# Twelve attention chunks ahead of two expert layers: the first four chunks in halves of 64 tokens

## The reference

```python
# q, k, v: (2, 8, 768, 64), block = 64
for b in range(nb):
    intra = np.einsum('bhic,bhjc->bhij', qb, kb) * Dmask[None]
    intra = np.einsum('bhij,bhjd->bhid', intra, vb)
    inter = np.einsum('bhid,bhde->bhie', qb * lam_pow[None], kv_state)
    out[:, :, sl] = intra + inter
    kb_dec = kb * rev_pow[None]
    kv_state = lam_block * kv_state + np.einsum('bhsd,bhse->bhde', kb_dec, vb)
x = out as (1536, 512)
h = x @ w_in;  g = np.maximum(0.01 * h, h);  x = g @ w_out
...
```

## Time and profile before

| | |
|---|---|
| median of 3 runs | 473.35 us (473.17 to 473.56) |
| the profiled execution: its own time | 473.61 us |
| its span, first to last instruction | 471.9 us |
| TensorE busy | 464.3 us, 98% of the span |
| VectorE, ScalarE, GpSimd busy | 42%, 36%, 43% |
| TensorE's share of the chain that ended last | 97% |
| first dense matmul starts | 21.50 us |
| mean rate of the DMA engines | 112 GB/s |

### The profile page before, as it was taken

One profiled execution on the slowest core, in us unless ns is written; L12 is line 12 of the kernel. 1 busy time (PEld: TensorE's weight loads), 2 busy tenths in 40 slices (PEclk: granted clock), 3 DMA queues, 4 the chain that ended last, 5 costly groups with the idle time before them and its releaser, 6 DMA issues.

```text
span 471.9 us, 9883 instructions
## 1 busy us (share of the span) xinstructions
PE 464.3 (98%) x3622; PEld 385.9 (82%) x3623; DVE 198.1 (42%) x467; ACT 168.9 (36%) x291; POOL 202.9 (43%) x207
## 2 busy tenths in 40 slices
PE   8899999999999999999999999999999999999996
PEld 5777777777778888887788888889999999999965
DVE  5643433344365522222472255668531455131212
ACT  2244334434453444444444465552111343111110
POOL 6875456455424456644444576513112325030102
PEclk9999999999999999999999999999999999999999
DMA  8884554430030450000760000131117878821101
GB/s 313 290 278 150 180 179 139 150 113 13 1 88 3 147 209 0 0 0 1 198 249 0 1 1 11 35 94 42 45 46 229 288 243 266 255 87 32 46 2 44
DMA packets 31185, 52.71 MB, mean 112 GB/s; under 512 B 8833, under 2 KB 19201, under 8 KB 31154
## 3 DMA queue, kind: packets, MB, share of 16 engines
q1 hardware_dynamic: 25808, 45.24, 29.5%
q0 software_dynamic: 2624, 7.03, 4.5%
q10 hardware_dynamic: 2722, 0.02, 0.3%
HBM read 45.87 MB, written 6.60 MB: 111 GB/s over the span
## 4 chain that ended last, share of the span: by engine, by line
PE 97%; DVE 1%; issue 1%; ACT 0%; POOL 0%; POOLq 0%; DVEq 0%
PE psum L1675 10%; PE psum L1685 9%; PE psum L1677 9%; PE psum L1676 9%; PE psum L1687 9%; PE psum L1686 9%; PE psum L1756 5%; PE psum L1757 5%; PE psum L1758 5%; PE psum L1772 5%; PE psum L1774 5%; PE psum L1773 5%; PE psum L1892 1%; PE psum L1520 1%; PE psum L1741 1%; PE psum L1619 1%
## 5 line engine op out<-in xcount | busy, mean ns | idle before, releaser
L677 POOL TENSOR_TENSOR wi_lo<-wd_raw,wi_hi 128x512 fp32r<-128x512 f32 x48 | 61.8, 1288 | 128.5 <-ACT wi_hi L863 128.4
L1675 PE MATMUL psum<-xT,wi_lo 128*128 128x512 f32 x192 | 77.4, 403 | 0.3 <-DVE xT L1113 0.3
L1685 PE MATMUL psum<-act_lo,wo_hi 128*128 128x512 f32 x192 | 75.7, 394 | 0.2 <-DVE act_lo L1176 0.2
L1677 PE MATMUL psum<-xT,wi_hi 128*128 128x512 f32 x192 | 75.0, 390 | 0.0
L1687 PE MATMUL psum<-act_hi,wo_hi 128*128 128x512 f32 x192 | 74.8, 390 | 0.0
L1676 PE MATMUL psum<-xT,wi_hi 128*128 128x512 f32 x192 | 74.8, 389 | 0.0
L1686 PE MATMUL psum<-act_hi,wo_lo 128*128 128x512 f32 x192 | 74.7, 389 | 0.0
L1173 DVE SCALAR_TENSOR_TENSOR act_f<-psum,act_f 128x512 f32<-128x512 f32 x48 | 33.1, 689 | 78.7 <-ACT act_f L884 78.3
L682 POOL TENSOR_TENSOR wo_lo<-wd_raw,wo_hi 128x512 fp32r<-128x512 f32 x48 | 61.9, 1290 | 4.1 <-ACT wo_hi L868 4.1
L884 ACT ACTIVATE act_f<-psum 128x512 f32<-128x512 f32 x48 | 28.7, 597 | 88.5 <-PE psum L1677 88.5
L1756 PE MATMUL psum<-xe_lo,we_hi 128*128 128x256 f32 x192 | 54.5, 284 | 0.0
(11 more groups left out here) (240 smaller groups left out, 735.8 us busy)
## 6 DMA issues: line engine op xcount, KB each, us to landing
we_raw<-w_exp SPq DMA_DIRECT2D x40, 512.0 KB, 5.3
qk_in<-attn_qk SPq DMA_DIRECT2D x10, 512.0 KB, 4.3
kv_in<-attn_kv SPq DMA_DIRECT2D x10, 512.0 KB, 3.3
wd_raw<-w_dense SPq DMA_DIRECT2D x16, 256.0 KB, 3.2
x_d<-x_r SPq DMA_DIRECT2D x12, 256.0 KB, 3.9
wd_raw<-w_dense SPq DMA_DIRECT2D x16, 128.0 KB, 2.9
wd_raw<-w_dense SPq DMA_DIRECT2D x32, 64.0 KB, 2.8
qk_more<-attn_qk SPq DMA_DIRECT2D x2, 512.0 KB, 5.7
```

The lines of the kernel that those rows point to most:

```text
L677: nc.gpsimd.tensor_tensor(wi_lo[:, r, :], dense_raw(f, 0), wi_hi[:, r, :].bitcast(F32), ALU.subtract).then_inc(s_wil, 1)
L1675: nc.tensor.matmul(h, w_lo, hi, start=(c == 0), stop=False)
L1677: mm = nc.tensor.matmul(h, w_hi, hi, start=False, stop=(c == DC - 1))
L1685: nc.tensor.matmul(bank(ACC + c), hi, act_lo[:, r, :], start=first, stop=False)
```

## The change

Chunks 0 to 3 take the half form too. What follows from that, engine by engine:

- **TensorE**: the old functions for whole chunks go. `early_scores`, `early_updates`, `early_values` and `early_state_part` are the half form, with a chunk's scores and then its output in the same two banks (`FIRST`) and updates in banks 6 and 7. The values come first and the state part adds to them; the second half of the values waits for the first half (`s_ho`). Chunk 0 has a state part for its second half alone. Seven warm-up matmuls stand in three places. The first `layer1` takes all products of the high parts first (`first_layer1`). The scores and updates of chunk 4 stand behind it.
- **VectorE**: mask and query decay of 64 columns; one operation per chunk for `probs`; a middle state (`early_middle`) and a next state of four small operations (`next_state`). The constants of the expert stage move behind the first pair of chunks.
- **ScalarE**: four products for the decayed state per chunk, which GpSimd made in one; the copies of the half mask go.
- **GpSimd**: key decay ahead of query decay; no state products; one more select in the setup; `wo_lo` of slice 0 behind the products for chunk 4.
- **SyncE**: keys and values ahead of queries from chunk 1 on; input weights of slices 0 and 1 together; queries and keys of chunk 4, then output weights of slices 0 and 1.

```diff
-WARM = (3, 5)
+WARM = (3, 2, 2)
+FIRST = (2, 4, 0, 2)
...
+            load_kv(1, 1)
             load_qk(1, 1)
-            load_kv(1, 1)
             sp.wait_ge(s_qk[0], 16)
+            load_kv(2, 2)
+            sp.wait_ge(s_kv[0], 16)
             load_qk(2, 2)
-            sp.wait_ge(s_kv[0], 16)
-            load_kv(2, 2)
+            sp.wait_ge(s_kv[1], 16)
+            load_kv(3, 3)
             sp.wait_ge(s_qk[1], 16)
             load_qk(3, 3)
-            sp.wait_ge(s_kv[1], 16)
-            load_kv(3, 3)
...
+            sp.wait_ge(s_qk[2], 16)
+            dense_in(0, s_wi[0])
+            sp.wait_ge(s_kv[3], 16)
+            dense_in(1, s_wi[1])
+            sp.wait_ge(s_qk[3], 16)
             next_qk(LEAD, 0, 0)
-            sp.wait_ge(s_qk[3], 16)
+            sp.wait_ge(s_wi[0], WLOAD - 16)
+            next_kv(LEAD, 0, 0)
+            sp.wait_ge(s_wi[1], WLOAD - 16)
             dense_out(0, 0)
-            sp.wait_ge(s_kv[3], 16)
-            dense_slice(1, 1, None)
-            sp.wait_ge(s_wi0, WLOAD - 16)
+            sp.wait_ge(s_qk[0], 32)
+            dense_out(1, 1)
+            sp.wait_ge(s_kv[0], 32)
             for u in range(2):
-                if u == 0:
-                    next_kv(LEAD, 0, 0)
-                    sp.wait_ge(s_qk[0], 32)
-                else:
+                if u == 1:
...
+            def decay_state(n):
+
+                act.wait_ge(s_st, n + 1)
+                for a in range(PAIRS):
+                    last = nc.scalar.activation(state_dec[:, a, :], start_state(n % 2)[:, a, :], ACT.Copy,
+                                                scale=q_decay[:, a, D - 1:D])
+                last.then_inc(s_sd, 1)
...
+            for n in range(1, LEAD):
+                decay_state(n)
+                attn(n - 1, out_bank(n - 1))
+            for f in range(2):
+                act.wait_ge(s_wi[f], WLOAD - 16)
+                act.sem_inc(s_wd[f], WLOAD - 16)
+                split_in(f, f, f, False)
+                if f == 0:
+                    attn(LEAD - 1, out_bank(LEAD - 1))
             act.wait_ge(s_wd[0], WLOAD)
             split_out(0, 0, 0, False)
             act.wait_ge(s_wd[1], WLOAD)
-            split_in(1, 1, 1, False)
```

```diff
+            nc.vector.tensor_copy(lam_b[:, 0:H], bank(0)[:, 0:H]).then_inc(s_lamb, 1)
             dve.wait_ge(s_lamb, 1)
             for h in range(H):
-                nc.vector.tensor_tensor_scan(decay_mask[:, h, :], lam_b[:, h:h + 1].broadcast_to([P, P + 1]), impulse[:], 0.0,
+                nc.vector.tensor_tensor_scan(decay_mask[:, h, :], lam_b[:, h:h + 1].broadcast_to([P, D]), impulse[:, 0:D], 0.0,
                                              ALU.mult, ALU.add).then_inc(s_mask, 1)
...
+            def next_state(n, u):
+
+                dve.wait_ge(s_mid, n + 1)
+                next_half(start_state(1 - u), state_mid[:, u], 1, s_st)
...
+            def early_middle(n):
+
+                dve.wait_ge(s_up, n + 3)
+                dve.wait_ge(s_sd, n)
+                nc.vector.tensor_tensor(state_mid[:, n % 2].rearrange("p a b -> p (a b)"), half_update_of(0),
+                                        state_dec[:].rearrange("p a b -> p (a b)"), ALU.add).then_inc(s_mid, 1)
+
             query_decay()
-            new_state(0, state_of(0), first=True)
-            scale(1, 1, score_bank(1))
+            dve.wait_ge(s_mask, H)
+            half_scale(0, 0, out_bank(0))
+            first_middle()
+            next_state(0, 0)
+            half_scale(1, 1, out_bank(1))
+            early_middle(1)
+            next_state(1, 1)
             chunk_lo(0, out_bank(0))
-            scale(2, 0, score_bank(2))
-            new_state(1, state_of(1))
+            early_middle(2)
+            half_scale(2, 0, out_bank(2))
+            next_state(2, 0)
+            half_scale(3, 1, out_bank(3))
+            early_middle(3)
             chunk_lo(1, out_bank(1))
-            scale(3, 1, score_bank(3))
-            state_by_halves(2)
+            dve.wait_ge(s_o, LEAD + 1)
+            next_state(3, 1)
             chunk_lo(2, out_bank(2))
```

```diff
+            def early_values(n):
+
+                pe.wait_ge(s_kv[n], 16)
+                pe.wait_ge(s_pr, 2 * n + 2)
+                half_values(n % 2, n, out_bank(n), True, first=True).then_inc(s_ho, 1)
+                pe.wait_ge(s_ho, n + 1)
+                half_values(n % 2, n, out_bank(n), False)
+
+            def early_state_part(n):
+
+                pe.wait_ge(s_qd, n + 1)
+                pe.wait_ge(s_mid, n + 1)
+                half_state_part(n, n % 2, out_bank(n), range(n == 0, 2), first=False).then_inc(s_o, 1)
+
+            def early_scores(n):
+
+                half_scores(n, n % 2, n, 16, out_bank(n))
+
+            def early_updates(n):
+
+                pe.wait_ge(s_st, n + 1)
+                half_updates(n, n % 2, n, 16)
...
+            early_scores(0)
+            warm(WARM[2])
+            early_updates(0)
+            early_values(0)
+            early_scores(1)
+            early_updates(1)
+            early_state_part(0)
+            early_values(1)
+            early_state_part(1)
+            early_updates(2)
+            early_scores(2)
+            early_values(2)
+            pe.wait_ge(s_xl, 3)
+            early_scores(3)
+            early_updates(3)
+            early_state_part(2)
+            early_values(3)
+            early_state_part(3)
...
+            def first_layer1():
+
+                h = bank(HID).rearrange("p (i n) -> p i n", i=TPB)
+                pe.wait_ge(s_wih, 1)
+                pe.wait_ge(s_xh, LEAD)
+                pe.wait_ge(s_xl, 4)
+                for c in range(DC):
+                    nc.tensor.matmul(h, wi_hi[:, 0, c * P:(c + 1) * P], xT[:, 0:TPB, 0, c, :], start=(c == 0), stop=False)
+                pe.wait_ge(s_wil, 1)
+                for c in range(DC):
+                    nc.tensor.matmul(h, wi_lo[:, 0, c * P:(c + 1) * P], xT[:, 0:TPB, 0, c, :], start=False, stop=False)
+                pe.wait_ge(s_xl, LEAD + 2)
+                for c in range(DC):
+                    mm = nc.tensor.matmul(h, wi_hi[:, 0, c * P:(c + 1) * P], xT[:, 0:TPB, 1, c, :], start=False, stop=(c == DC - 1))
                 mm.then_inc(s_l1, 1)
...
+            first_layer1()
...
+                    pe.wait_ge(s_xl, c + 2)
+                    half_scores(c, u, u, 16 * m, 6)
+                    half_updates(c, u, u, 16 * m)
+                    layer1(n + 1, 1, 0)
+                    layer2(n, 0, first=first and u == 0)
+                    state_and_values(c, u, last=last and u == 1)
                     if last and u == 1:
                         return
-                    layer1(n + 2, 0, 0, between=(c, u, True))
+                    layer1(n + 2, 0, 0, between=(c, u))
```

More of the change, by code:

```diff
@@ L360, in fused_program @@
         s_wd = [sem(f"dense_weights_loaded{f}") for f in range(WSEM)]
-        s_wi0 = sem("first_slice_wi_loaded")
+        s_wi = [sem(f"first_slices_wi_loaded{f}") for f in range(2)]
         s_wih = sem("wi_hi_ready")
@@ L1344, in chunk_pair @@
                     chunk_lo(c, 6)
-            chunk_pair(2, reset=True, first=True)
+            chunk_pair(2, reset=True)
+            constants()
             with dve.Fori(3, 5) as m:
@@ L1578, in half_scores @@
-            def half_scores(n, u, loaded):
-                pe.wait_ge(s_qk[u], loaded)
-                pe.sem_inc(s_pass, 1)
-                for h in range(H):
-                    rows = slice((h % 2) * D, (h % 2 + 1) * D)
                     for s in range(2):
-                        mm = nc.tensor.matmul(half_scores_of(h)[half_rows(s)], qk_of(u)[rows, 1, h // 2, half_rows(s)],
-                                              qk_of(u)[rows, 0, h // 2, s * D:(s + 1) * D], start=True, stop=True)
+                        mm = nc.tensor.matmul(half_scores_of(b, h)[half_rows(s)], qk_of(slot)[rows, 1, h // 2, half_rows(s)],
+                                              qk_of(slot)[rows, 0, h // 2, s * D:(s + 1) * D], start=True, stop=True)
@@ L1613, in half_state_part @@
                 pe.sem_inc(s_pass, 1)
-                for s in range(2):
-                    frm = state_mid if s else start_state(u)
-                    for i in range(2):
-                        for h in (2 * i, 4 + 2 * i, 5 + 2 * i, 1 + 2 * i):
-                            rows = slice((h % 2) * D, (h % 2 + 1) * D)
-                            nc.tensor.matmul(out_at(6, h)[:, s * D:(s + 1) * D], frm[rows, h // 2, :],
-                                             q_dec[rows, u, h // 2, s * D:(s + 1) * D], start=(s == 0 and i == 0), stop=False,
-                                             skip_group_check=True)
@@ L1634, in attend, with turned_values @@
[L1634 to L1638 removed]
+                half_state_part(n, u, 6)
+                half_values(u, u, 6, False).then_inc(s_ho, 1)
+            def turned_values(n, u):
+                pe.wait_ge(s_ho, n + 1)
+                pe.sem_inc(s_pass, 1)
```

(3 more changed lines are left out.)

320 lines of the change are left out of this document (84 added, 236 removed).

## The result

The changed kernel takes 480.61 us (480.00 to 480.93, four runs) against 473.46 for the kernel before beside it (473.17 to 474.65, four runs). The ratio is 1.0145 with a 95% interval of 1.0124 to 1.0165. It is **7.15 us slower**, where 2.2 us faster was forecast. The profiled execution took 480.93 us, with a span of 479.2.

A forecast was written before the change was run, and what follows sets the result against it. TensorE, busy almost without gap after 21.50 us, was taken as the bound, so only an earlier dense start helps: 2.9 - 0.47 (chunk 4 scores) - 0.2 (late weights) = 2.2 us, giving 471.1 us, range 470.0 to 473.0.

The forecast's parts named there:

- the path, "step by step": TensorE's lead-in over chunks 1 to 3, from 9.25 us: dense start at 18.6 us, 2.9 us earlier than before.
- It doubles the instructions of three of the four parts: Half form of a chunk on TensorE: more instructions at smaller pitch, 2.33 us for 3.15, saving 0.82 us a chunk.
- the wait for the first half of a chunk's values: New TensorE wait before the second half of values, three times on the path: under 0.1 us each, nearer nothing.
- Rival 4: Lead-in chunks: quarter tiles save nothing, a chunk stays at 3.15 us, 2.5 us missing, 473.6 us; chance 0.05.
- Rival 1: TensorE lead-in: clock stays at 1.2 GHz longer, 472.1 us (low through chunk 1) or 475.1 (chunk 2 too); chance 0.12.
- the old kernel's pause ahead of 21.50 us did not slow what followed: Argument against the low clock: the wait before the old dense start left the following work at full speed.
- Scores of chunk 1: TensorE lead-in: with the new transfer order they start at about 9.25 us, against 9.6 before.
- the scans: Chunk 0: eight scans, cut from 129 to 64 columns, take 0.2 us each, 1.6 in all, against 2.65.
- The 0.47 us for the scores behind the start: Chunk 4's scores now follow the dense start: scores and updates, 0.62 + 0.47, replace one 0.62 us group; 0.47 lost.
- Rival 2: Dense start: input weights of slice 0 or output weights of slice 1 land late, 1.2 us lost, 472.3; chance 0.14.
- ScalarE's four products: Decayed state in the lead-in chunks: 0.2 us each, 0.8 us together, ahead of the middle state.
- rival 3: Lead-in state chain sets the pace: ScalarE products at 0.35 us each cost 0.6 in two chunks, 472.3; chance 0.09.

The follow-up runs named there:

- the bf16 runs: Changed kernel, chunks 0 to 3 reading upper halves of fp32 operands as bf16, without or with 25, 31, 41 filler matmuls: ratios 0.9992, 0.9990, 1.0001, 0.9999.
- the bf16 kernel: Changed kernel with matmuls of chunks 0 to 3 reading only the upper halves of their fp32 operands, as bf16, no filler matmuls: 473.13 us, ratio 0.9992.
- the first experiment: Changed kernel with SyncE holding the queries of chunk 4 and all transfers behind them until the update of chunk 3 is done: 476.88 us, ratio 1.0083.
- the fourth experiment: Kernel before with only the changed kernel's order of the first dense group, high-part products first: 472.88 us, ratio 0.9996.
- the seventh experiment: Kernel before with 24 TensorE semaphore instructions ahead of the values of chunk 3: 478.47 us, ratio 1.0099.
- the second experiment: Changed kernel with sixteen unused 32-column matmuls between the values of chunk 0 and the scores of chunk 1: 481.33 us (one run).

## Why the prediction was wrong

**The failed step** is the path, "step by step", from 9.25 us to a dense start at 18.6. It let TensorE issue the moment its data was there. "It doubles the instructions of three of the four parts" stood in the text, but was priced only in pitch (14.7 to 19.4 ns an instruction, measured in chunks that come one in 14 us, between dense groups). In a row, the chunks want a block of 256 every 2.3 us, and the trace has 5.2, 4.4 and 6.0 us from one block to the next (8.10, 13.27, 17.68, 23.63). That is 4.8 us of stops in the chain (0.80, 0.69, 3.27), where the sum had none.

The start came 7.1 us late in all (25.67), so the stops are not the whole. A second term was mis-sized: the wait for the first half of a chunk's values, taken at "under 0.1 each" and nearer to nothing. The second half started 0.54 us after the first in each of the three chunks (11.48 to 12.02, 16.01 to 16.55, 19.48 to 20.02), where sixteen rows of the same size without a wait need 0.24 (those of a state part, 18.79 to 19.03). That is 0.3 each, 0.9 us together. Another 0.8 us was lost ahead of the values of chunk 1 (11.48 for 10.65), with the clock low over its scores, and 0.3 in the last state part, behind the fall (0.82 for 0.48).

Rival 4 had the right suspicion, no gain from more instructions, by the wrong mechanism. At 2.4 GHz its 25 ns do not occur: the score rows of chunks 2 and 3 took 0.54 and 0.48 us for 32, 15 to 17 ns each.

**Rival 1**, the low clock, came true, but not by its cause or place. It looked for a rise later than about 12 us; the rise was at 10.33, and the chunks from the updates of chunk 1 on ran at 2.4 GHz until the clock fell behind the 3.27 us stop, for the first dense group: 2.4 us. In the bf16 runs it is low over that group without any stop. The argument against it, that "the old kernel's pause ahead of 21.50 us did not slow what followed", was drawn from 0.34 us.

**What held.** Scores of chunk 1 started at 9.40 (9.25 forecast), the scans took 0.2 each (1.57 for eight), and the first probabilities ran from 6.66. In the bf16 kernel, without the stops, the dense start came at 17.45, ahead of the 18.6. That does not prove the rest of the path, as TensorE had half the instructions there. The 0.47 us for the scores behind the start came as priced (0.62 and 0.47 against one group of 0.62). Rival 2 did not come: TensorE did not wait for weights.

**What was off in size.** ScalarE's four products took 1.06 us (0.27 each) against 0.8, the near side of rival 3. In the bf16 runs it shows as the 1.59 us wait ahead of the values of chunk 2, whose probabilities stand behind the middle state on VectorE.

**Not tried:** the new order of transfers alone, and chunks in halves for only some of the four.

## What to carry to other kernels

Count instructions, not only columns: splitting an fp32 matmul in two adds four instructions, and where many short ones follow each other, TensorE can outrun the fetch of its own program. Here a block of 256 took 4.0 us to come with no data moving and up to 6.0 with data in its way. In a profile this shows as "issue" stops in the middle of a group, at equal counts, each ended 2.3 to 2.6 us after a packet on the instruction queue; look for one in the kernel before, where a single stop of 0.6 us is the sign that the limit is near, and in more than one execution, because it comes and goes. And a cost measured in isolated groups is no price for the same groups back to back.

## What the runs showed of the hardware that was not expected

- From the entering of a block to the start of the next fetch it took 2.0 to 3.7 us in the changed kernel, with data moving, and 1.8 us with none moving (the first experiment). With the DMA engines 97% busy or more it was anything from 1.3 us (the fourth experiment) to 4.7 (the kernel before), so load alone does not set it.
- A TensorE semaphore instruction took 0.14 us (94 of them 13.14 us).
- A stop of 3.3 to 3.5 us brought the clock to 1.2 GHz for 6.8 us (23.98 to 30.80 after the change, 20.50 to 27.33 in the seventh experiment). The first dense group paid 2.4 us for it after the change. In the seventh it paid 0.8 (3.63 us, 25.68 to 29.31), since there most of the low stretch lay over the chunk's own matmuls. In the bf16 lead-in, made of quarter tiles, the clock fell behind waits of 2.1, 0.9 and 0.5 us.
- With the same TensorE program up to there, the clock rose at 6.61 us (the second experiment), 8.05 (the first) and 10.33 (the changed kernel).
